# Zero rows of the routed token table: six tiles per expert written from stage 29 instead of one tile per expert after the last stage, with the first expert's weight split two stages earlier

## The chip, the cores and the metric

The kernel runs on one core of a Trainium2 chip. The metric is the device time of one execution in microseconds, 1207.06 us as the median of three runs (1206.76 to 1207.32). The core has a matrix engine (PE), two elementwise engines (DVE and ACT), a general engine (POOL) that also issues transfers, and SP, which only issues transfers. The engines meet through semaphores. Each engine runs its own instructions in the order in which they are written.

## The reference, cut to what matters

```
attn = softmax over the scores that lie within tau of the row's maximum, times v     # 4 batches x 8 heads, 576 rows, 64 columns
x    = attn as 2304 rows of 512
e    = argmax over 8 experts of cosine(x, expert_emb)
x2   = gate * (relu(x @ w1[e]) @ w2[e])                # each row by its own expert only, F = 1024
out  = softplus(x2 @ w_in) @ w_out                     # 512 -> 2048 -> 512
```

Which rows go to which expert is known only while the kernel runs, so the rows are regrouped by expert in a table in DRAM.

## The kernel before

The program has three blocks, one after the other, with a barrier of all engines between them.

**Attention** runs `stages(step)`, 36 stages numbered -1 to 34, on every engine. Stage i works on several heads at once, out of phase: in stage i PE computes the scores of head i+1 for the row maxima (`scores`), the transposed scores of head i-1 (`scores_T`), and the products with v of heads i-2 and i-1 (`values`). In stage i it also transposes the row maxima of head i (`max_T`), which the POOL makes ready in `max_lo(i)`, and the output of head i-2 (`out_T`). Each stage of a POOL program is: `write_x`, which normalises a finished head into the rows `XF` and `XR`; `q_lo` and `k_lo`, the low parts of q and k two heads ahead; `max_lo`; then the weight work of `split_first`; then the scatters. SP's stage is: q and k of head i+4, once the buffers are free, then v of head i+1 into the one of two v buffers that head i-1 has left (`sp.wait_ge(s_pv, TILES * (n - 1))`, n = i+1). SP's wait makes its stage i run while PE is already in stage i+1. The last head is 31, and its v is requested in SP's stage 30 and first read by PE in stage 32, in `values(32, 6)`, which waits on `s_vin`.

**The routed table.** After a batch's eighth head its expert choices are made (`choose_a`, `choose_b`), ranked on PE (`rank`) and turned into row numbers (`places`), and the POOL scatters the batch's 576 rows of 512 numbers into `xs_dram` with five indirect transfers. Expert e owns the rows from e*CAP on, filled from the bottom; `rt.base` is the next free row of each expert. The experts block later reads the table in tiles of 128 rows (slots), so a last, partly filled tile would read rows that nobody wrote. Hence the kernel zeroes rows. At SP's stage 2 it zeroes the 7 tiles behind the last expert. After the last stage it reads the eight final ends from `tail_row` and zeroes one tile of 128 rows from each of them (L304 to L310), then waits until all nine fills have landed, and with that the attention block ends on SP.

**The first expert's weights.** At SP's stage 4 two transfers of 2 MB fetch w1[0] and w2[0] into `first[0]` and `first[1]` (semaphore `s_e0`). At POOL's stage 7 `split_first` waits for both and issues two more transfers that copy them, converted, into the ring. In stages 9 to 12 and 16 to 19 the POOL computes the low parts, a quarter of a matrix per stage (`SPLITS`).

**The end of the block on PE** is the last `rank`, then 26 matmuls whose results nobody reads (`warm_up`).

**Experts** starts with 9 such matmuls on PE, then `x_T(0, 0)`, the transposes of the first tile, and `up(0, 0)`. The first tile is loaded by SP (L938) once all scatters have landed. ACT first computes the sums of squares of the last batch, a square root and an exponential (L1107, L1109), and then `x_hi`, the high part of the transposed tile; DVE computes the gates and then `x_lo` (L1205), for which `up` waits. From here on each tile is a slot, 25 of them, and **last_layer** follows.

Of the kernel before, what the change touches and what calls it, by code (L numbers as in the profile page):

```python
# [12 lines left out]
P = 128  # L13
B, H, S, D = 4, 8, 576, 64
# [5 lines left out]
N = B * S  # L20
DM = H * D
TT = N // P
E, F1 = 8, 1024
# [5 lines left out]
BANK = 512  # L29
# [1 line left out]
HALF = S // 2  # L31
TILES = 2 * CH
QUARTER = KD * F1
CAP = N + P
WORK = 45568


# [32 lines left out]
def warm_up(nc, out, src, times):  # L70


    for _ in range(times):
        nc.tensor.matmul(out, src[:, 0:P], src[:, 0:BANK], start=True, stop=True)

class Routing:

# [21 lines left out]
def attention(nc, sem, pb, areas, ident, XF, XR, raw, ring, first, rt, emb_en, qT, kT, v, tau, emb, moe_tau, w1, w2, xs_dram):  # L99
# [37 lines left out]
    tail_row = ar("tail_row", [1, E], I32)  # L137
    zeros = ar("zeros", [P, DM // 2], F32)
# [19 lines left out]
    sc_ps = pb("sc_ps", [P, 2 * BANK], F32)  # L158
# [14 lines left out]
    def unit(q):  # L173

        return ring[:, 0, q, :]
# [42 lines left out]
    s_tail = sem("s_tail")  # L218
    s_zero = sem("s_zero")
# [16 lines left out]
    def batch_end(b):  # L236

        return H * b + H + 2

    def batch_at(i, steps):  # L240

        b, off = divmod(i - batch_end(0) - steps, H)
        return b if off == 0 and 0 <= b < B - 1 else None
# [20 lines left out]
    with block:  # L264
        @block.sync
        def _(sp):
            sp.dma_start(emb_sb[:, :], emb).then_inc(s_emb, 16)
            for h in range(2):
                load_twice(sp, q_in[h], q_h, h, s_qin[h])
                load_twice(sp, k_in[h], k_h, h, s_kin[h])  # L270
                if h == 0:
                    sp.dma_start(tau_b[:, :], tau.partition_broadcast(P)).then_inc(s_tau, 16)
            sp.dma_start(tau2_b[:, :], moe_tau.partition_broadcast(E)).then_inc(s_tau2, 16)
            load_v(sp, v1[0], 0, s_vin[0])

            def next_q_k(i):
                n = i + 4
                if live(n):
                    sp.wait_ge(s_qlo, n - 1)
                    load_twice(sp, q_in[n % 2], q_h, n, s_qin[n % 2])  # L280
                    sp.wait_ge(s_klo, n - 1)
                    sp.wait_ge(s_kh1, n - 1)
                    load_twice(sp, k_in[n % 2], k_h, n, s_kin[n % 2])

            def step(i):
                next_q_k(i)
                n = i + 1
                if n >= 1 and live(n):
                    if n >= 2:
                        sp.wait_ge(s_pv, TILES * (n - 1))  # L290
                    load_v(sp, v1[n % 2], n, s_vin[n % 2])
                if i == 4:
                    sp.dma_start(first[0][:, :].rearrange("p (kc f) -> p kc f", f=F1),
                                 w1[0].rearrange("(kc p) f -> p kc f", p=P)).then_inc(s_e0, 16)
                    sp.dma_start(first[1][:, :].rearrange("p (kc d) -> p kc d", d=DM),
                                 w2[0].rearrange("(kc p) d -> p kc d", p=P)).then_inc(s_e0, 16)

                if i == 2:
                    sp.wait_ge(s_con, CONSTS)
                    sp.dma_start(xs_dram[E * CAP:E * CAP + (E - 1) * P, :].rearrange("(p s) (h d) -> p (s h) d", p=P, h=2),  # L300
                                 zeros[:, :].unsqueeze(1).to_broadcast([P, 2 * (E - 1), DM // 2])).then_inc(s_zero, 16)

            next_q_k(-2)
            stages(step)  # L304

            sp.wait_ge(s_tail, 1)
            for e in range(E):
                at = sp.value_load(tail_row[0:1, e:e + 1], min_val=0, max_val=E * CAP - P)
                sp.dma_start(xs_dram[bass.ds(at, P), :].rearrange("p (h d) -> p h d", h=2),
                             zeros[:, :].unsqueeze(1).to_broadcast([P, 2, DM // 2])).then_inc(s_zero, 16)  # L310
            sp.wait_ge(s_zero, 16 * (E + 1))

        @block.tensor
        def _(pe):
# [123 lines left out]
            pe.wait_ge(s_ones, 1)  # L438
            stages(step)
            rank(B - 1)  # L440
            pe.wait_ge(rt.s_w[0], 1)
            warm_up(nc, sc_ps[:, 0:BANK], unit(0), 26)

        @block.scalar
        def _(act):
# [95 lines left out]
        def _(dve):  # L541
# [86 lines left out]
            def places(b):  # L628
                dve.wait_ge(s_rk, b + 1)
                base, after = rt.base[b % 2], rt.base[(b + 1) % 2]  # L630
                nc.vector.tensor_tensor(after[:, :], rank_ps[:, CH * E:(CH + 1) * E], base[:, :],
                                        ALU.add).then_inc(s_rkr, 1)
                nc.vector.tensor_tensor(pl[:, :, :], rank_ps[:, 0:CH * E].rearrange("p (c e) -> p c e", e=E),
                                        base[:, :].unsqueeze(1).to_broadcast(wide), ALU.add).then_inc(s_rkr, 1)
                dve.wait_ge(s_rkr, 2 * (b + 1))
                link(nc.vector.tensor_tensor(pl[:, :, :], pl[:, :, :], oh[:, 0:CH, :].bitcast(F32), ALU.mult))
                link(nc.vector.reduce_sum(plf[:, :], pl[:, :, :], AX_X))
                nc.vector.tensor_copy(rt.place[:, b, :], plf[:, :]).then_inc(s_place, 1)

            def tables():  # L640
# [8 lines left out]
                link(nc.vector.reduce_sum(se[:, :], pre[:, :, :], AX_X))  # L649
                nc.vector.tensor_scalar(rt.step[:, :], nsl[:, :], -float(P), float(CAP), ALU.mult, ALU.add)  # L650
                link(nc.vector.tensor_tensor(past[:, :, :],
# [11 lines left out]
            def step(i):  # L663
                for k in range(CH):
                    row_max(i, k)
                    if k == 0:
                        rden_(i)
                    mask(i, k)
                    if i == 0 and k == 3:
                        emb_rows()  # L670
                    if i == 1 and k == 0:
                        emb_cols()
                    if k == 1 and batch_at(i, 1) is not None:
                        choose_a(batch_at(i, 1))
                    if k == 3 and batch_at(i, 1) is not None:
                        choose_b(batch_at(i, 1))
                    if k == 1 and batch_at(i, 2) is not None:
                        places(batch_at(i, 2))

            for t in kh1:  # L680
                nc.vector.memset(t[D:96, 0:S].bitcast(F32), 1.0)
# [10 lines left out]
            choose_a(B - 1)  # L692
            choose_b(B - 1)
            places(B - 1)
            nc.vector.tensor_copy(tail_row[:, :], rt.base[B % 2][0:1, :]).then_inc(s_tail, 1)
            tables()

        @block.gpsimd
        def _(pool):
# [95 lines left out]
                                        ALU.mult).then_inc(s_x, 1)  # L795

            def scatter(b, chunks):
                pool.wait_ge(s_place, b + 1)
                pool.wait_ge(s_x, X_OPS * H * (b + 1))
                for c in chunks:  # L800
                    rows = P if c < FULL else REM
                    src = XF[:, b % 2, c, :] if c < FULL else XR[0:REM, b % 2, :]
                    pool.indirect_dma_start(xs_dram, bass.IndirectOffsetOnAxis(rt.place[0:rows, b, c:c + 1], 0),
                                            src, None).then_inc(s_scat, 16)
                    scattered[0] += 1

            SPLITS = {9: (0, 0), 10: (0, 1), 11: (0, 2), 12: (0, 3), 16: (1, 0), 17: (1, 1), 18: (1, 2), 19: (1, 3)}

            def split_first(i):

                if i == 7:
                    pool.wait_ge(s_e0, 32)
                    for u in range(2):
                        pool.dma_start(unit(2 * u), first[u][:, :]).then_inc(rt.s_cast[u], 16)
                if i == 20:
                    pool.dma_start(raw[0][:, :].rearrange("p (kc f) -> p kc f", f=F1),
                                   w1[1].rearrange("(kc p) f -> p kc f", p=P)).then_inc(rt.s_raw[0], 16)
                if i in SPLITS:
                    u, c = SPLITS[i]
                    pool.wait_ge(rt.s_cast[u], 16)  # L820
                    part = QUARTER // 4
                    w = slice(c * part, (c + 1) * part)
                    ins = nc.gpsimd.tensor_tensor(unit(2 * u + 1)[:, w], first[u][:, w],
                                                  unit(2 * u)[:, w].bitcast(F32), ALU.subtract)
                    if c == 3:
                        ins.then_inc(rt.s_w[u], 1)
# [31 lines left out]
def experts(nc, sem, pb, start, ident, XF, XR, raw, ring, rt, gate, dest, w1, w2, w_in, w_out, xs_dram, ys_dram):  # L858
# [26 lines left out]
    h_ps = [pb(f"b_h{i}", [P, BANK], F32) for i in range(2)]  # L885
    ht_ps = [pb(f"b_ht{i}", [P, BANK], F32) for i in range(2)]
    y_ps = pb("b_y", [P, BANK], F32)
    wu_ps = pb("b_wu", [P, BANK], F32)
# [32 lines left out]
    with nc.Block() as block:  # L921
# [107 lines left out]
        def _(pe):  # L1029
# [48 lines left out]
                    ins = nc.tensor.matmul(y_ps[:, :], htl[:, kc, :], hi, start=False, stop=kc == KF1 - 1)  # L1078
                ins.then_inc(s_y, 1)

            warm_up(nc, wu_ps[:, :], ring[:, 0, 0, :], 9)
            x_T(0, 0)
            up(0, 0)
            pe.wait_ge(rt.s_tab, 1)
# [151 lines left out]
def last_layer(nc, sem, pb, start, ident, ring, raw, gate, dest, ys_dram, out):  # L1236
# [25 lines left out]
    h_ps = [pb(f"c_h{i}", [P, BANK], F32) for i in range(2)]  # L1262
# [42 lines left out]
    with nc.Block() as block:  # L1305
# [53 lines left out]
        def _(pe):  # L1359
# [42 lines left out]
                    ins = nc.tensor.matmul(o_ps[t][:, :], g_lo, w_hi, start=False, stop=fc == KF2 - 1)  # L1402
                ins.then_inc(s_l2, 1)

            warm_up(nc, h_ps[0][:, :], ring[:, 0, 0, :], 12)
            for c in range(FULL):
                tile_T(0, c, yg_first[:, c, :])

# [222 lines left out]
```

## Time and profile before

| | |
|---|---|
| median of three runs | 1207.06 us |
| the profiled execution | 1207.06 us, its span 1205.1 us, so 1.96 us lie outside the span |
| PE busy | 1148.0 us, 95% of the span |
| DVE, ACT, POOL busy | 49%, 45%, 39% |
| transfers of SP (queue q1) | 49.58 MB in 45376 packets |
| transfers of the POOL (queue q0) | 84.94 MB in 14496 packets |

The span is the time from the first instruction to the last. PE is the engine that is nearly always busy. PE idles mostly at the start, and at the border between attention and experts. The granted clock of PE, printed as PEclk, is 1.00 at 2.4 GHz and 0.50 at 1.2 GHz; over the span it is 0.985.

### The profile page before, as it was taken

The page shows a single profiled execution, that of the slowest core. Times are in us where ns is not written, and L with a number is a line of the kernel's source. Part 1 is how long each engine was busy: PE and PEld are TensorE (multiplying, and loading weights), DVE is VectorE, ACT ScalarE, POOL GpSimd, SP SyncE. Part 2 cuts the span into 40 slices and gives each one's busy share as a digit, 9 for nine tenths or more (in the row PEclk, how much of TensorE's full clock was granted, in tenths as well). Part 3 has the DMA queues.
Part 4 walks back from the last instruction along what each step waited for, and adds up shares of the span by engine and source line. Part 5 has one row for each costly group of instructions (what it writes and reads, how often), then busy time and mean ns, then how long its engine had stood idle before and what let it go on. Part 6 is the DMA issues. An engine that isn't in the chain of part 4 may idle for free. (4 is left out here: it accounts for less than half of the span.)

```text
span 1205.1 us, 17818 instructions
## 1 busy us (share of the span) xinstructions
PE 1148.0 (95%) x5875; PEld 939.5 (78%) x5876; DVE 586.3 (49%) x991; ACT 544.5 (45%) x997; POOL 465.8 (39%) x476
## 2 busy tenths in 40 slices
PE   3999999999999859999999999699999999999997
PEld 2888888888888647888888888578788788878886
DVE  3666676676666322221222212375565655655554
ACT  3566666656665422222222222454444544544454
POOL 4333454554333127257645566123213213223121
PEclk9999999999999969999999999999999999999999
DMA  3148413124211066776778767300000000000000
GB/s 103 51 139 267 133 51 113 50 79 150 79 51 50 10 209 242 236 255 242 267 257 313 257 234 244 123 1 27 10 35 27 9 35 17 17 35 19 1 36 18
DMA packets 59935, 135.32 MB, mean 112 GB/s; under 512 B 24280, under 2 KB 28120, under 8 KB 57056
## 3 DMA queue, kind: packets, MB, share of 16 engines
q0 software_dynamic: 14496, 84.94, 20.2%
q1 hardware_dynamic: 45376, 49.58, 13.9%
q8 instruction: 35, 0.57, 0.2%
q14 instruction: 28, 0.23, 0.1%
HBM read 76.83 MB, written 19.92 MB: 80 GB/s over the span
## 5 line engine op out<-in xcount | busy, mean ns | idle before, releaser
L1354 POOL TENSOR_TENSOR gl<-rc,gh 128x512 fp32r<-128x512 f32 (+1 forms) x80 | 92.9, 1181 | 300.5 <-ACT gh L1482 300.5
L358 PE MATMUL out_ps<-pT,v 128*66 128x288 f32 x640 | 187.1, 407 | 2.1 <-ACT oT L479 1.3
L569 DVE TENSOR_REDUCE mx<-sc_ps 128x1 f32<-128x576 f32 x160 | 121.2, 758 | 137.3 <-PE sc_ps L320 131.6
L974 POOL TENSOR_TENSOR ring<-raw,ring 128x1024 f32 (+1 forms) x64 | 151.0, 2397 | 46.3 <-DMA ring<-raw 46.1
L455 ACT ACTIVATE ering<-st_ps,esc 128x576 f32<-128x576 f32 x160 | 118.4, 740 | 45.9 <-PE st_ps L320 35.1
L579 DVE SCALAR_TENSOR_TENSOR pT<-st_ps,thr,ering 128x576 f32<-128x576 f32 x160 | 128.5, 803 | 7.4 <-ACT ering L455 7.4
L1385 PE MATMUL c_h<-c_xT,ring 128*128 128x512 f32 (+2 forms) x320 | 120.8, 377 | 3.0 <-DVE c_xT L1506 3.0
L1386 PE MATMUL c_h<-c_xT,ring 128*128 128x512 f32 (+2 forms) x320 | 120.8, 378 | 0.0
L319 PE MATMUL st_ps<-qhh,khl 128*128 128x288 f32 x320 | 119.6, 389 | 0.0
L1387 PE MATMUL c_h<-c_xT,ring 128*128 128x512 f32 (+2 forms) x320 | 119.6, 374 | 0.0
L1532 DVE TENSOR_SCALAR rc<-c_h 128x512 f32<-128x512 f32 (+1 forms) x80 | 51.0, 637 | 137.4 <-ACT ea L1469 135.8
L1400 PE MATMUL c_o<-ring,gh 128*128 128x512 f32 x288 | 115.5, 401 | 1.3 <-POOL gl L1354 1.3
L319 PE MATMUL sc_ps<-khl,qhh 128*128 128x288 f32 x320 | 96.1, 315 | 20.1 <-DVE identr L690 14.6
L1401 PE MATMUL c_o<-ring,gh 128*128 128x512 f32 x288 | 114.0, 396 | 0.0
L1402 PE MATMUL c_o<-ring,gl 128*128 128x512 f32 x288 | 114.0, 396 | 0.0
L1469 ACT ACTIVATE ea<-c_h 128x512 f32<-128x512 f32 (+1 forms) x80 | 44.4, 555 | 151.1 <-PE c_h L1387 151.1
L358 PEld LDWEIGHTS out_ps<-pT,v 128*66 128x66 f32 x640 | 83.4, 137 | 33.1 <-ACT oT L479 4.2
L1216 DVE TENSOR_TENSOR htl<-b_ht,hth 128x512 fp32r<-128x512 f32 x50 | 32.2, 686 | 131.8 <-ACT hth L1123 131.8
L320 PE MATMUL sc_ps<-khl,qlm 128*128 128x288 f32 x320 | 92.6, 303 | 0.0
L320 PE MATMUL st_ps<-qlm,kh 128*128 128x288 f32 x320 | 90.4, 297 | 0.0
L1052 PE MATMUL b_h<-ring,xth 128*128 (+1 forms) x200 | 82.6, 413 | 4.9 <-DVE xtl L1205 4.3
L1076 PE MATMUL b_y<-ring,hth 128*128 x200 | 81.2, 406 | 1.9 <-DVE htl L1216 1.9
(201 smaller groups left out, 2331.3 us busy)
## 6 DMA issues: line engine op xcount, KB each, us to landing
ring<-raw POOLq DMA_DIRECT2D x16, 2048.0 KB, 10.3
raw<-in_moe_w_dram POOLq DMA_DIRECT2D x14, 2048.0 KB, 9.6
q_in<-in_q_dram SPq DMA_DIRECT2D x64, 144.0 KB
k_in<-in_k_dram SPq DMA_DIRECT2D x64, 144.0 KB, 2.9
xs<-rows_in SPq DMA_DIRECT2D x25, 256.0 KB, 3.9
slots_out<-ys SPq DMA_DIRECT2D x25, 256.0 KB, 4.0
v<-in_v_dram SPq DMA_DIRECT2D x32, 128.0 KB
first<-in_moe_w_dram SPq DMA_DIRECT2D x2, 2048.0 KB, 11.6
```

Source lines behind the costliest of these rows:

```text
L319: nc.tensor.matmul(out[:, h, :], stat1[:, w], mov1[:, m], start=True, stop=False)
L320: ins = nc.tensor.matmul(out[:, h, :], stat2[:, w], mov2[:, m], start=False, stop=True)
L358: nc.tensor.matmul(out_ps[0:VW, 0:HALF], v1[n % 2][:, c, :], pT[n % 2][c][:, h * HALF:(h + 1) * HALF], start=c == 0, stop=c == CH - 1).the ...
L455: nc.scalar.activation(flat(ering[b]), halves(st_ps[b]), ACT.Exp, scale=esc[:, :]).then_inc(s_e, 1)
L569: nc.vector.reduce_max(mx[n % 2][:, c:c + 1], halves(sc_ps), AX_XY).then_inc(s_max, 1)
L579: nc.vector.scalar_tensor_tensor(out=flat(pT[n % 2][c]), in0=halves(st_ps[t % 2]), scalar=thr[:, :], in1=flat(ering[t % 2]), op0=ALU.is_ge ...
L974: ins = nc.gpsimd.tensor_tensor(ring[:, bass.ds(side, 1), 2 * u + 1, w].rearrange("p o w -> p (o w)"), raw[u][:, w], ring[:, bass.ds(side, ...
L1385: nc.tensor.matmul(h_ps[fc % 2][:, 0:n], w_hi, x_hi, start=kc == 0, stop=False)
L1386: nc.tensor.matmul(h_ps[fc % 2][:, 0:n], w_hi, x_lo, start=False, stop=False)
L1387: ins = nc.tensor.matmul(h_ps[fc % 2][:, 0:n], w_lo, x_hi, start=False, stop=kc == KD - 1)
L1400: nc.tensor.matmul(o_ps[t][:, :], g_hi, w_hi, start=fc == 0, stop=False)
L1401: nc.tensor.matmul(o_ps[t][:, :], g_hi, w_lo, start=False, stop=False)
```

## The change

- `CAP`, the rows that each expert owns, goes from 2432 to 3 * 576 + 6 * 128 = 2496, so the tables' addresses shift.
- `tail_row` is now copied from `rt.base` after batch 2's places (in DVE's stage 28), and holds where batch 3 will begin for each expert. In SP's stage 29, behind the load of head 30's v, eight fills of 768 rows each (1536 pieces of 1 KB, 1.57 MB per fill, 12.58 MB in all) are issued. They cover whatever rows batch 3 will take (at most 576) and one tile beyond. The eight fills of 128 rows after the last stage are gone, the final wait for all nine stays.
- Since batch 3's rows are now written over zeroed rows, the POOL waits for the fills before it scatters batch 3.
- The 26 unread matmuls at the end of attention are gone, and those at the start of experts go from 9 to 24.
- `split_first` waits for `s_e0` and issues its two transfers in stage 5 instead of 7; the quarters are computed in stages 7 to 12 and 16, 17.

```diff
-CAP = N + P
+TAIL = 6
+CAP = 3 * S + TAIL * P
...
+                if i == batch_end(B - 2) + 3:
+
+                    sp.wait_ge(s_tail, 1)
+                    for e in range(E):
+                        at = sp.value_load(tail_row[0:1, e:e + 1], min_val=0, max_val=E * CAP - TAIL * P)
+                        sp.dma_start(xs_dram[bass.ds(at, TAIL * P), :].rearrange("(p s) (h d) -> p (s h) d", p=P, h=2),
+                                     zeros[:, :].unsqueeze(1).to_broadcast([P, 2 * TAIL, DM // 2])).then_inc(s_zero, 16)
...
-            sp.wait_ge(s_tail, 1)
-            for e in range(E):
-                at = sp.value_load(tail_row[0:1, e:e + 1], min_val=0, max_val=E * CAP - P)
-                sp.dma_start(xs_dram[bass.ds(at, P), :].rearrange("p (h d) -> p h d", h=2),
-                             zeros[:, :].unsqueeze(1).to_broadcast([P, 2, DM // 2])).then_inc(s_zero, 16)
             sp.wait_ge(s_zero, 16 * (E + 1))
...
-            pe.wait_ge(rt.s_w[0], 1)
-            warm_up(nc, sc_ps[:, 0:BANK], unit(0), 26)
...
+                        if batch_at(i, 2) == B - 2:
+                            nc.vector.tensor_copy(tail_row[:, :], rt.base[(B - 1) % 2][0:1, :]).then_inc(s_tail, 1)
...
-            nc.vector.tensor_copy(tail_row[:, :], rt.base[B % 2][0:1, :]).then_inc(s_tail, 1)
...
             def scatter(b, chunks):
+                if b == B - 1:
+                    pool.wait_ge(s_zero, 16 * (E + 1))
...
-            SPLITS = {9: (0, 0), 10: (0, 1), 11: (0, 2), 12: (0, 3), 16: (1, 0), 17: (1, 1), 18: (1, 2), 19: (1, 3)}
+            SPLITS = {7: (0, 0), 8: (0, 1), 9: (0, 2), 10: (0, 3), 11: (1, 0), 12: (1, 1), 16: (1, 2), 17: (1, 3)}
...
-                if i == 7:
+                if i == 5:
                     pool.wait_ge(s_e0, 32)
...
-            warm_up(nc, wu_ps[:, :], ring[:, 0, 0, :], 9)
+            warm_up(nc, wu_ps, ring[:, 0, 0, :], 24)
```

What stands in a row on SP around the end of attention. The numbers behind `v` tell its two buffers apart; the last `v_79` is head 31's. Before:

```order
L259 DMA v_78<-in_v_dram 128x4x64 [waits s_pv]
L261 DMA v_78<-in_v_dram 64x64
L259 DMA v_79<-in_v_dram 128x4x64 [waits s_pv]
L261 DMA v_79<-in_v_dram 64x64
L308 TENSOR_LOAD tail_row [waits s_tail]
L308 ISA x2
L309 ISA
L309 DMA rows_in<-zeros 256x1x256
```

Of the eight fills after the change, the first and the last are shown:

```order
L260 DMA v_78<-in_v_dram 128x4x64 [waits s_pv]
L262 DMA v_78<-in_v_dram 64x64
L307 TENSOR_LOAD tail_row [waits s_tail]
L307 ISA x2
L308 ISA
L308 DMA rows_in<-zeros 1536x1x256
...
L308 DMA rows_in<-zeros 1536x1x256
L260 DMA v_79<-in_v_dram 128x4x64 [waits s_pv]
L262 DMA v_79<-in_v_dram 64x64
L265 UNCONDITIONAL_BRANCH [waits s_zero]
```

All eight fills now stand ahead of the load of head 31's v on the one queue.

On the POOL, around the copies of the first expert's weights. `mt<-mx` is `max_lo`, `khl` the end of `k_lo`. Before, in stages 6 and 7:

```order
L773 TENSOR_TENSOR mt<-mx_116,mt 128x5 [waits s_mhi]
L765 TENSOR_TENSOR khl_131<-k_in_74,khl_131 64x576 [waits s_mt,s_qlo,s_khi]
L788 TENSOR_TENSOR LP_88<-os_82,rden_114 128x5x8 [waits s_rd,s_klo]
L790 TENSOR_TENSOR XF<-os_82,rden_114 128x4x64
L793 TENSOR_TENSOR XR<-os_82,rden_114 64x64
L751 TENSOR_TENSOR qlm_128<-q_in_73,qhh_124 128x576 [waits s_qhh]
L773 TENSOR_TENSOR mt<-mx_117,mt 128x5 [waits s_mhi]
L765 TENSOR_TENSOR khl_132<-k_in_75,khl_132 64x576 [waits s_mt,s_qlo,s_khi]
L814 DMA ring<-first_69 128x4096 [waits s_e0,s_klo]
L814 DMA ring<-first_70 128x4096
```

After, at the end of stage 5 and in stage 6:

```order
L774 TENSOR_TENSOR mt<-mx_117,mt 128x5 [waits s_mhi]
L766 TENSOR_TENSOR khl_134<-k_in_75,khl_134 64x576 [waits s_mt,s_qlo,s_khi]
L817 DMA ring<-first_69 128x4096 [waits s_e0,s_klo]
L817 DMA ring<-first_70 128x4096
L789 TENSOR_TENSOR LP_88<-os_83,rden_115 128x5x8 [waits s_rd]
L791 TENSOR_TENSOR XF<-os_83,rden_115 128x4x64
L794 TENSOR_TENSOR XR<-os_83,rden_115 64x64
L752 TENSOR_TENSOR qlm_127<-q_in_72,qhh_123 128x576 [waits s_qhh]
L774 TENSOR_TENSOR mt<-mx_116,mt 128x5 [waits s_mhi]
```

The wait for `s_e0` moved from behind stage 7's `max_lo` to ahead of stage 6's.

On PE, at the border of the blocks, before:

```order
L412 MATMUL tr_ps<-oh,ones_sq 128x8
L74 MATMUL sc_ps<-ring 128x512 [waits s_w0]
L74 MATMUL sc_ps<-ring 128x512 x25
L264 UNCONDITIONAL_BRANCH
L1028 UNCONDITIONAL_BRANCH [waits barrier_Pool_Activation_PE_DVE_SP_release]
L74 MATMUL b_wu<-ring 128x512 x9
L1036 MATMUL b_tr<-ident,xs_6229 128x128 [waits s_xs0]
```

and after:

```order
L414 MATMUL tr_ps<-oh,ones_sq 128x8
L265 UNCONDITIONAL_BRANCH
L1031 UNCONDITIONAL_BRANCH [waits barrier_Pool_Activation_PE_DVE_SP_release]
L75 MATMUL b_wu<-ring 128x512 x24
L1039 MATMUL b_tr<-ident,xs_6203 128x128 [waits s_xs0]
```

The unread matmuls now all stand behind the barrier.

## Rows read from the trace of the kernel before

**Rows 1.** Busy time by stretch: from:to, length, engines, PEclk, DMA share, GB/s.
```profile
50.00:373.00 323.00, 322.92 (x2042) 271.30 (x2041) 210.03 (x330) 208.94 (x398) 140.97 (x182) 1.00 0.37 106
```

**Rows 2.** Order of time: start, us, engine, line, operation [idle before <-releaser]. The border.
```profile
422.73 0.17 DVE L638 CAST place<-plf 128x5 int32<-128x5 f32 x1
423.18 1.03 POOL L803 DMA_INDIRECT rows_in<-XF,place  x1 [3.87 <-DVE place L638]
423.97 11.54 SPq L309 DMA_DIRECT2D rows_in<-zeros  x8
428.31 0.90 POOL L803 DMA_INDIRECT rows_in<-XR,place  x1 [0.30 <-issue]
437.86 4.18 PE L74 MATMUL b_wu<-ring 128*128 128x512 f32 x9 [8.00 <-PEq L264]
```

**Rows 3.** Order of time, SP around its stage 4.
```profile
86.65 0.59 SPq L293 DMA_DIRECT2D first<-in_moe_w_dram  x1
87.28 0.51 SPq L295 DMA_DIRECT2D first<-in_moe_w_dram  x1
92.34 1.18 SPq L256 DMA_DIRECT2D k_in<-in_k_dram  x2
```

**Rows 4.** The tile `first`: from issue to landing of SP's two transfers.
```profile
DMA to landing us min/median/max: 8.4/11.6/14.8
```

**Rows 5.** The tile `k_in`: to landing, those issued at 92.34, then those of 76.12.
```profile
DMA to landing us min/median/max: 10.4/10.7/11.1
...
DMA to landing us min/median/max: 2.8/2.9/3.0
```

**Rows 6.** Order of time, POOL's stages 5 to 7.
```profile
85.48 1.43 POOL L765 TENSOR_TENSOR khl<-k_in,khl 64x576 fp32r<-64x576 f32 x1 [0.17 <-POOL mt L773]
...
93.91 0.26 POOL L788 TENSOR_TENSOR LP<-os,rden 128x40 f32<-128x40 f32 x1 [7.00 <-DVE rden L591]
...
96.98 0.20 POOL L773 TENSOR_TENSOR mt<-mx,mt 128x5 fp32r<-128x5 f32 x1 [0.61 <-ACT mt L463]
...
110.98 1.35 POOL L814 DMA_DIRECT2D ring<-first  x2 [0.31 <-POOL khl L765]
```

**Rows 7.** Order of time, PE: max_T of stage 6.
```profile
99.17 0.77 PE L374 MATMUL tr_ps<-identr,mt 128*128 128x128 f32 x4
```

**Rows 8.** Busy time by stretch: during the fill issued at 62.91, the loads of `first`, the border.
```profile
65.00:66.00 1.00, 1.00 (x8) 0.79 (x7) 0.41 (x1) 0.95 (x3) 0.00 (x0) 1.00 1.02 351
66.00:67.00 1.00, 1.00 (x10) 0.84 (x8) 1.00 (x2) 0.05 (x1) 0.00 (x0) 1.00 1.04 347
...
90.00:95.00 5.00, 5.00 (x35) 4.34 (x34) 2.80 (x6) 3.28 (x6) 1.09 (x4) 1.00 1.01 372
...
430.00:436.00 6.00, 0.00 (x0) 0.00 (x0) 0.00 (x0) 0.00 (x0) 0.00 (x0) 0.73 0.69 217
```

**Rows 9.** Order of time, SP: v of head 30, then of head 31.
```profile
385.79 0.37 SPq L259 DMA_DIRECT2D v<-in_v_dram  x1
386.21 0.52 SPq L261 DMA_DIRECT2D v<-in_v_dram  x1
...
397.18 0.37 SPq L259 DMA_DIRECT2D v<-in_v_dram  x1
```

**Rows 10.** Order of time, PE: values(32, 6) and what follows, and the 26 unread matmuls.
```profile
407.76 1.16 PE L358 MATMUL out_ps<-pT,v 128*66 128x288 f32 x4
...
420.72 1.21 PE L412 MATMUL tr_ps<-oh,ones_sq 128*128 128x40 f32 x5
421.78 8.08 PE L74 MATMUL sc_ps<-ring 128*128 128x512 f32 x26
```

**Rows 11.** PE by stretch: length, PE busy (instructions), PEclk, DMA share, GB/s.
```profile
419.00:420.00 1.00, 0.00 (x0) 0.53 0.00 0
...
425.00:426.00 1.00, 1.00 (x4) 0.55 0.93 341
426.00:427.00 1.00, 1.00 (x6) 1.00 0.88 314
...
453.00:454.00 1.00, 1.00 (x6) 0.90 1.18 475
```

**Rows 12.** Order of time, start of experts.
```profile
445.27 0.58 ACT L1113 ACTIVATE xth<-b_tr 128x512 fp32r<-128x512 f32 x1
446.43 0.68 DVE L1205 TENSOR_TENSOR xtl<-b_tr,xth 128x512 fp32r<-128x512 f32 x1
447.16 0.80 PE L1052 MATMUL b_h<-ring,xth 128*128 128x512 f32 x1 [4.26 <-DVE xtl L1205]
```

More of the change, by code:

```diff
@@ L73, in warm_up @@
     for _ in range(times):
-        nc.tensor.matmul(out, src[:, 0:P], src[:, 0:BANK], start=True, stop=True)
+        nc.tensor.matmul(out[:, :], src[:, 0:P], src[:, 0:BANK], start=True, stop=True)
 class Routing:
@@ L1403, in second @@
                 ins.then_inc(s_l2, 1)
-            warm_up(nc, h_ps[0][:, :], ring[:, 0, 0, :], 12)
+            warm_up(nc, h_ps[0], ring[:, 0, 0, :], 12)
             for c in range(FULL):
```

## The prediction

> **What bounds the kernel now.** I read the busy time by stretch first. Through attention PE is busy 322.92 us of 323 [rows 1], so whatever holds PE there is added to the time in full; no other engine can win it back. Then I read the order of time at the border of attention and experts. The last batch's row numbers are ready at 422.90, the POOL's five scatters run from 423.18 to 429.21, but experts start only at 437.86, and PE idles 8.00 us [rows 2]. What ends last there is SP, whose eight fills are issued over 11.54 us from 423.97 and must land. This is what the change takes away. Last I looked at where the moved work goes: SP's and POOL's rows around stage 4 to 7 and stage 29 to 32 [rows 3 to 7, 9, 10], and the rates of the transfers [rows 8].
>
> **Part 1: the POOL's wait in stage 5.** SP issues the two 2 MB loads of `first` at 86.65 and 87.28 [rows 3]. They land 8.4 and 14.8 us later [rows 4], the second at 87.28 + 14.8 = 102.1. Before, the POOL asks at 110.98 [rows 6] and waits for nothing. After, it asks when stage 5's `k_lo` is done, at 85.48 + 1.43 = 86.9, and stands until 102.1. Queued behind it on the POOL are the two copies (0.3 to start and 1.35, [rows 6]) and stage 6: from the start of `LP` at 93.91 to the start of `mt` at 96.98 it is 3.07 us, of which 0.61 was waiting, so 2.46 of work, then 0.20 for `mt`, and 0.3 to get going. `mt` is then done at 102.1 + 1.65 + 0.3 + 2.46 + 0.20 = 106.7, where it was 97.18. PE needs it for `max_T` at 99.17 [rows 7] and is held 7.5 us; everything behind on PE (the scores, the products) waits too.
>
> PE has then been idle that long, and the clock matters. In the rows the granted clock falls to 0.53 in the slice 419 to 420, after idle time, and after work has started again (PE's row at 420.72, the rank's matmuls) it is back at 1.00 only from about 425.9; from the start at 447.16 it stays low until about 453.2 [rows 10 to 12]. That is 5.2 to 6.0 us at 1.2 GHz instead of 2.4, of which about half is lost where PE is the bound: I take 2.7 us. Part 1 costs 7.5 + 2.7 = 10.2 us. Its lower end is 7.5, should the other engines' waits hide the slow clock; its upper end 11.
>
> The copies now run beside the loads of q and k for head 10, as they ran beside those of head 11; that collision cost PE nothing before (the whole of rows 1), so 0, at most 2 if ACT is caught. The quarters of `SPLITS` are the same eight instructions, in stages where the POOL idles 7.00 us [rows 6]: 0. They and the weights are ready by stage 17, long before they are used: 0. The new `CAP` changes only addresses: 0.
>
> **Part 2: the fills on SP's queue.** The first fill follows head 30's v, whose second load ends its issue at 386.21 + 0.52 = 386.73 [rows 9]. `tail_row` has been ready since stage 28, so SP doesn't wait. A fill of the same form (pieces of 1 KB) moves 351 and 347 GB/s in whole microseconds [rows 8]; 12.58 MB take 12.58 / 0.349 = 36.0 us. Batch 2's last three scatters (0.66 MB) share the engines, 1.9 us. With 1.3 us until the first bytes flow, the fills end at 386.73 + 1.3 + 36.0 + 1.9 = 425.9.
>
> Behind them in the queue stands head 31's v, issued at 397.18 before [rows 9]. That SP's queue works in order shows at stage 4: the small `k_in` loads issued at 92.34, behind the 4 MB, took 10.4 to 11.1 us to land, against 2.8 to 3.0 without such a load ahead [rows 5]; they landed 1.2 us after `first`. So v lands at about 425.9 + 0.4 + 1.2 = 427.5. PE wants it at 407.76 [rows 10] and is held 19.7 us, and after that it runs slow for a while, again 2.7. For the fill rate I keep both ends: 372 GB/s, as the load of `first` [rows 8], makes the hold 2.2 us shorter, and 314 GB/s, the slice 426 to 427 [rows 11] with fills and scatters mixed, 4.1 us longer.
>
> The Trainium skill ("DMA: Bandwidth & Descriptors", "Where 436 GB/s comes from") gives about 358 GB/s as what a core gets of the DRAM. By that figure the fill would take 35.1 us and the time would be 0.9 us less. The 372 GB/s of the stretch 90 to 95 [rows 8] go past it, so I leave it out of the sum.
>
> **Part 3: the border.** All of it moves by 19.7 + 2.7 = 22.4. The last scatter's issue ends at 428.31 + 0.90 + 22.4 = 451.6. The fills are then long in, so the wait that the POOL has been given is free, and SP has only the wait for them left, also done. With 0.3 for the barrier experts start at 451.9, against 437.86: +14.0 (without the hold it would be 429.5, and this part would win 8.3).
>
> At the start of experts, PE now has 24 unread matmuls. The 26 took 8.08 us [rows 10], low until 425.9 and full after: 0.43 and 0.24 us each fit that. From an idle start, 5.3 us low do 12 of them, the other 12 take 2.9, together 8.2 us. ACT's path to `xth` takes 445.27 - 437.86 = 7.4 us [rows 2, 12], and the first tile must wait for the scatters' landing and its own load, which I put at 5 to 6 us, so the unread matmuls are now what ends last. Then come four transposes (0.6), `xth` 0.58, `xtl` 0.68 and the handovers, 2.1 in all: `up` starts 10.3 us into the block, against 447.16 - 437.86 = 9.3 [rows 12]: +1.0. In return `up` finds the clock high: the low stretch from 447.16 to 453.2 is gone, -2.7 (taken as above; 0 if the short idle time before `up` lets the clock fall again).
>
> **The sum.** 10.2 + 14.0 + 1.0 - 2.7 = +22.5 us. Later PE is the bound again and the POOL's weight copies move with the block, so nothing more is won or lost. The profiled execution took 1207.06 us (1205.1 span and 1.96 around it), which is also the median: 1229.6 us, with a span near 1227.6. Its own range is 1222 to 1238: down by 2.2 for the rate, 2.7 for the clock in part 1 and 2.7 more for part 2's, up by 4.1 and by 2.7 and 2 for the clock and ACT.
>
> **The rivals.**
>
> *Head 31's v isn't late.* Its transfer overtakes the fills. For it: it is a separate, small transfer. Against: the landing times [rows 5]. Then only the POOL waits, for the fills until about 427 instead of starting at 423.18: the border moves 3.8 later than without them, experts start at 433.3, `up` at 443.6, -3.6 and -2.7 for the clock, +10.2 of part 1: 1211.0. In the Trainium skill ("DMA: Bandwidth & Descriptors", "Queues, rings and completion order") completion is not in order per issuing engine, but each ring's entries are taken in order; that lends this rival little.
>
> *The wait in stage 5 doesn't reach PE.* Part 1 is 0, the rest stays: 1219.4. Against it: PE needs `mt` 2.0 us after the POOL has it [rows 6, 7], and the POOL is 15.2 us late.
>
> *The shorter border decides.* The place is the end of SP's work at 437.86, its price up to -8.3, +1.0 and -2.7, -10.0 in all, and it decides as long as what the two queues hold PE is less than 10.0 us together. With no hold on PE and only the POOL's wait of 3.8, the time is 1200.8. For it: this stretch holds 8.00 us of idle PE [rows 2], surely on the path. Against: part 1 alone uses it up.
>
> *The fills run slower than I think.* Eight small fills moved only 217 GB/s in 430 to 436 [rows 8]. At that rate 12.58 MB take 58.0 us, 22.0 more: 1251.6. Against: those were bound by their issue, 1.5 us for each 256 KB, and the large fill was not.
>
> **Chances.** My forecast 0.75; v in time 0.07; stage 5 hidden 0.06; the shorter border 0.04; slow fills 0.08. The range 1210 to 1244 leaves out the last two. A change of 0.2%, 2.4 us, is about what a measurement of this kernel can tell from none. Faster by more than that comes from the fourth case: 0.04, and 0.01 for what I haven't thought of; same 0.02, between the cases; slower 0.93.
>
> **What the profile after would show.** Part 1: POOL idle for about 15 us from 86.9, ended by the landing of `first`, PE idle 7.5 us before the `max_T` that stood at 99.17, then the clock at half for 5 to 6 us. Part 2: SP's issue of the fills drawn out over some 30 us, and PE idle about 20 us before a `values` matmul, ended by the landing of v; PEclk low behind it. Part 3: no idle SP time between the last scatter and the barrier, 24 matmuls over 8.2 us, and `up` at full clock. I am wrong if PE doesn't wait for v, or if the transfers in that stretch stay well off 349 GB/s.

## The result and the profile after

The changed kernel takes 1234.35 us (median of four runs, 1233.67 to 1235.82), the kernel before 1206.91: ratio 1.0228, interval 1.021 to 1.0246, so 27.4 us slower. The forecast was 1229.6. The profiled execution took 1232.68 us with a span of 1230.8, which is 25.7 us more than the span before; the comparison below is of these two.

What PE waited for in the changed kernel, longest first (engine, line, waited for: us in total, times, longest):

```profile
PE out_ps L360 <- DMA v<-in_v_dram: 21.6, 1, 21.6
PE sc_ps L321 <- DVE identr L692: 14.7, 1, 14.7
PE b_wu L75 <- PEq L265: 10.7, 1, 10.7
PE tr_ps L376 <- POOL mt L774: 6.4, 1, 6.4
```

The first and the fourth are new. The second is the program's start, the third the border between the blocks, which was 8.0 long before [rows 2]. The same two holds in order of time (start, duration, engine, and in brackets the wait before it):

```profile
85.14 1.43 POOL L766 TENSOR_TENSOR khl<-k_in,khl 64x576 fp32r<-64x576 f32 x1 [0.17 <-POOL mt L774]
101.58 1.35 POOL L817 DMA_DIRECT2D ring<-first  x2 [15.01 <-DMA first<-in_moe_w_dram]
...
105.39 0.19 POOL L774 TENSOR_TENSOR mt<-mx,mt 128x5 fp32r<-128x5 f32 x1
...
105.63 1.12 PE L376 MATMUL tr_ps<-identr,mt 128*128 128x128 f32 x4 [6.42 <-POOL mt L774]
...
394.66 0.52 SPq L262 DMA_DIRECT2D v<-in_v_dram  x1
396.46 30.66 SPq L308 DMA_DIRECT2D rows_in<-zeros  x8
427.16 4.54 SPq L260 DMA_DIRECT2D v<-in_v_dram  x1
437.69 2.16 PE L360 MATMUL out_ps<-pT,v 128*66 128x288 f32 x4 [21.56 <-DMA v<-in_v_dram]
```

The POOL stands 15.01 us behind its `k_lo`, its `mt` comes at 105.39 instead of 96.98 [rows 6], and `max_T` at 105.63 instead of 99.17 [rows 7]. SP stands in the issue of the eight fills for 30.66 us (the first two of them alone take 2.04 us in e5_spread below), and v is requested only at 427.16 instead of 397.18 [rows 9]. PE's `values(32, 6)` starts at 437.69 instead of 407.76 [rows 10].

The border of the blocks, in order of time:

```profile
452.41 1.21 PE L414 MATMUL tr_ps<-oh,ones_sq 128*128 128x40 f32 x5
460.49 0.90 POOL L806 DMA_INDIRECT rows_in<-XR,place  x1 [0.30 <-issue]
464.35 7.75 PE L75 MATMUL b_wu<-ring 128*128 128x512 f32 x24 [10.73 <-PEq L265]
...
471.94 0.60 PE L1039 MATMUL b_tr<-ident,xs 128*128 128x128 f32 x4
473.95 0.50 PE L1055 MATMUL b_h<-ring,xth 128*128 128x512 f32 x1 [1.41 <-DVE xtl L1208]
```

The last scatter's issue ends at 461.39, and yet experts start only at 464.35. The rows of the barrier's line say why: what each queue did there (operation, duration in ns, start). Changed kernel:

```profile
L265 SPq DRAIN  x1: 7/7/7, 437.1 to 437.1; - x1
L265 PEldq DRAIN  x1: 1477/1477/1477, 452.2 to 452.2; - x1
L265 POOLq DRAIN  x1: 7041/7041/7041, 457.0 to 457.0; - x1
```

and before:

```profile
L264 POOLq DRAIN  x1: 10645/10645/10645, 423.0 to 423.0; - x1
L264 SPq DRAIN  x1: 7/7/7, 437.6 to 437.6; - x1
```

In both kernels experts start 0.2 to 0.3 us after the last of these drains has ended. The POOL's drain (its row starts at 457.03) ends at 464.1, 2.7 us behind its last issue. Before it ended at 433.6, and SP, at 437.6, was later by 4.0.

Last, PE around the end of experts, by stretch (length, PE busy, PEclk, DMA share, GB/s). Changed:

```profile
784.00:786.00 2.00, 1.24 (x5) 1.00 0.43 159
786.00:788.00 2.00, 2.00 (x6) 0.52 0.00 0
788.00:790.00 2.00, 2.00 (x7) 0.63 0.00 0
```

Before:

```profile
760.00:762.00 2.00, 0.82 (x4) 1.00 0.57 217
762.00:764.00 2.00, 2.00 (x10) 1.00 0.06 12
```

Behind the same idle time of 1.88 us (PE waits for `htl` there in both) the clock falls to half for about 3 us in one and not in the other.

| place | before | changed | later by |
|---|---|---|---|
| max_T of stage 31 | 398.51 | 406.94 | 8.4 |
| rank (its ones_sq matmuls) | 420.72 | 452.41 | 31.7 |
| experts start | 437.86 | 464.35 | 26.5 |
| up starts | 447.16 | 473.95 | 26.8 |
| first hidden transposes | 456.63 | 480.71 | 24.1 |
| last hidden transposes | 758.26 | 781.84 | 23.6 |
| last layer starts | 770.26 | 795.39 | 25.1 |
| end | 1205.1 | 1230.8 | 25.7 |

### The profile page after: what moved, and what is told of

It is laid out like the page before. It is cut to its first block and busy times, and to the rows that moved or that the text cites. A ratio compares the mean times of both kernels' runs of the same rounds, so it can differ in the third digit from the quotient of the medians.

```text
span 1230.8 us, 17795 instructions
## 1 busy us (share of the span) xinstructions
PE 1146.4 (93%) x5864; PEld 937.6 (76%) x5865; DVE 585.5 (48%) x991; ACT 545.1 (44%) x997; POOL 466.2 (38%) x476
## 5 line engine op out<-in xcount | busy, mean ns | idle before, releaser
L360 PE MATMUL out_ps<-pT,v 128*66 128x288 f32 x640 | 189.2, 411 | 23.5 <-DMA v<-in_v_dram 21.6
L789 POOL TENSOR_TENSOR LP<-os,rden 128x40 f32<-128x40 f32 x32 | 8.2, 255 | 198.3 <-DVE rden L591 198.2
```

The source lines that it names most:

```text
L360: nc.tensor.matmul(out_ps[0:VW, 0:HALF], v1[n % 2][:, c, :], pT[n % 2][c][:, h * HALF:(h + 1) * HALF], start=c == 0, stop=c == CH - 1).the ...
```

## The experiments

The theory: two queues hold PE, one after the other. The POOL stands in stage 5 until `first` has landed, and v stands in SP's queue behind 12.58 MB of fills. The rivals are that slack hides the first, that the load on the 16 transfer engines rather than the order in the queue holds v, and that the number of the fills, not their bytes, costs the time.

**e1_split_only**, the kernel before with the weight work moved and nothing else:

```diff
-SPLITS = {9: (0, 0), 10: (0, 1), ... 19: (1, 3)}
+SPLITS = {7: (0, 0), 8: (0, 1), 9: (0, 2), 10: (0, 3), 11: (1, 0), 12: (1, 1), 16: (1, 2), 17: (1, 3)}
-                if i == 7:
+                if i == 5:
                     pool.wait_ge(s_e0, 32)
```

> The kernel before with only the move of the first expert's weight work: the wait for s_e0 and the two copies in stage 5 instead of 7, the quarters in stages 7 to 12 and 16, 17. Theory (the POOL stands until the second load of first has landed, and PE behind it): POOL idle about 15 us, PE held 6.5 to 7 us before max_T of stage 6, then some 5 us at half clock that cost 2 more, so +8.8 us on the kernel before, 1215.7. Rival (the hold is taken up by slack in later stages and the loss of the changed kernel is all in the fills): +0 to +3 us, under 1210.

Measured: 1216.99 us, ratio 1.0082 (1.0066 to 1.0099), so 10.3 more than the kernel before. In its trace the POOL stands 15.55 us, PE waits once for `mt`:

```profile
PE tr_ps L374 <- POOL mt L773: 7.0, 1, 7.0
```

`max_T` of stage 31 is 9.9 us late (408.39), and the end of experts shows the slow clock again (13.5 us from the last transposes to the last layer, 12.0 before). The hold in stage 5 reaches PE, and later stages don't make up for it. The rival falls.

**e2_old_split**, the changed kernel with that move undone (the diff above, reversed).

> The changed kernel with the wait for s_e0, the copies and the quarters back in their old stages; fills, row capacity and unread matmuls stay changed. Theory (the two holds on PE are separate and add up): 8.8 us less than the changed kernel's 1234.35, so 1225.5, with PE still held 21 to 22 us for head 31's v. Rival (the hold in stage 5 shifts something that the fills would otherwise hit anyway, so that the holds overlap): less than 5 us gained, over 1229.

Measured: 1224.14 us, ratio 1.0146 (1.0129 to 1.0163). The wait for v is as long as in the changed kernel, and the one for `mt` is gone from PE's list:

```profile
PE out_ps L360 <- DMA v<-in_v_dram: 21.5, 1, 21.5
```

The parts add up: 10.3 + 17.4 = 27.7 against 27.4 for both.

**e3_v_on_act**, the changed kernel with head 31's v issued from ACT's queue:

```diff
+                        if i == HEADS - 1:
+                            load_v(act, v1[i % 2], i, s_vin[i % 2])     # ACT's stage, behind out_copy(i, 1)
...
-                if n >= 1 and live(n): ... load_v(sp, v1[n % 2], n, s_vin[n % 2])
+                (the same for n < HEADS - 1 only)
```

> The changed kernel, but the two transfers of head 31's v are issued from ACT's own queue, in its stage 31 behind the out_copy that already waits for the same buffer to be free. Theory A (v was late because it stood behind 12.58 MB in SP's queue): v is issued near 406 and lands within 3 to 14 us (k_in took 13.4 us beside the POOL's copies), PE is held 0 to 4 us at values(32, 6) instead of 21.6. Then the POOL's new wait decides: the row numbers are ready near 431, the fills land near 437, so the scatters start 18 us earlier than in the changed kernel: about 1216. Theory B (the 16 transfer engines are full, and whichever queue v is in it lands only when the fills are through): PE held about 20 us, 1232 to 1235.

Measured: 1216.59 us, ratio 1.0077 (1.0054 to 1.01). In order of time, ACT's issue and the POOL's first scatter:

```profile
405.89 0.44 ACTq L260 DMA_DIRECT2D v<-in_v_dram  x1
406.37 1.60 ACTq L262 DMA_DIRECT2D v<-in_v_dram  x1
...
437.04 1.03 POOL L809 DMA_INDIRECT rows_in<-XF,place  x1 [8.25 <-DMA rows_in<-zeros]
```

PE doesn't wait for v at all, though all eight fills are under way beside it (SP issues them over 30.70 us from 396.73, as in the changed kernel). So it was the order in one queue, not the load of the engines. The other expected wait takes its place: the POOL idles 8.25 us until the fills have landed, the last 4.7 of them with the row numbers ready (`place` is done at 432.38). The Trainium skill ("DMA: Bandwidth & Descriptors", "Issuing engines are not separate DMA queues") says that transfers of different issuers run on the same 16 engines and interleave, and that several issuers save only issue time. The trace agrees with the interleaving. It doesn't agree that only issue time is at stake: for this one small transfer the choice of the issuer was worth 17.8 us of the kernel's time, since on SP the fills stood ahead of it.

**e4_three_tiles**, half the bytes per fill (the upper three tiles of each expert's range aren't zeroed):

```diff
-xs_dram[bass.ds(at, TAIL * P), :] ... [P, 2 * TAIL, DM // 2]
+xs_dram[bass.ds(at, 3 * P), :] ... [P, 2 * 3, DM // 2]
```

> The changed kernel with fills of 3 tiles (384 rows) instead of 6, so 6.29 MB in all. It leaves out the zeroing of the upper three tiles of each expert's range; with these inputs batch 3 gives no expert that many rows. Theory (the hold is the fills' bytes over their rate, 341 GB/s in the changed kernel): fills through 18.4 us earlier, v lands near 419.5, PE held about 3.5 us instead of 21.6, and most of the slow clock behind it goes too: 1215 to 1217. Rival (the hold is mostly issue cost on SP, eight issues with their register reads, whatever their size): still held over 12 us, over 1225.

Measured: 1213.66 us, ratio 1.0071 (1.0049 to 1.0093). The hold, in order of time:

```profile
395.91 14.31 SPq L308 DMA_DIRECT2D rows_in<-zeros  x8
410.26 2.55 SPq L260 DMA_DIRECT2D v<-in_v_dram  x1
418.56 1.16 PE L360 MATMUL out_ps<-pT,v 128*66 128x288 f32 x4 [2.97 <-DMA v<-in_v_dram]
```

Half the bytes take 18.6 us off the hold, 6.29 MB at 338 GB/s. The same eight issues with the same register reads cost PE at most these 2.97 us. The time is a little better than expected; the hold was 0.5 us shorter than the 3.5 put for it. The clock does fall behind it, but not for long: it reads 0.50 in 420 to 422 and 0.84 in 422 to 426.

**e5_spread**: with what was learned, the fills are spread so that at most two stand between two loads of v, and the weight work is back in its stages:

```diff
-                if i == batch_end(B - 2) + 3:
+                FILLS = {batch_end(B - 2) + 2: (0, 1), batch_end(B - 2) + 3: (2, 3), batch_end(B - 2) + 4: (4, 5, 6, 7)}
+                if i in FILLS:
                     sp.wait_ge(s_tail, 1)
-                    for e in range(E):
+                    for e in FILLS[i]:
```

> The changed kernel with the first expert's weight work back in its old stages, and the eight fills split over three of SP's stages: experts 0 and 1 in stage 28, 2 and 3 in stage 29, 4 to 7 in stage 30, each time behind that stage's load of v. Theory (fills cost time only by standing ahead of v, 4.6 us for each 1.57 MB): at most two fills, 9.2 us, stand between one v and the next, 11.9 us later, the last four end near 418, before the row numbers at 422.9; no hold. The last scatter is issued by 429.2, the POOL's drain ends 2.7 us later, experts start near 432.1 instead of 437.9, up starts at 441.7 at full clock: 8 us less than the kernel before, 1198.7 (1197.5 to 1200). Rival (12.58 MB of writes beside attention and the scatters cost time wherever they are): no faster than 1205.

Measured: 1200.94 us, ratio 0.9956 (0.9943 to 0.9968): faster than the kernel before, by 5 us instead of 8. In order of time:

```profile
388.22 2.04 SPq L308 DMA_DIRECT2D rows_in<-zeros  x2
396.67 0.39 SPq L260 DMA_DIRECT2D v<-in_v_dram  x1
...
399.15 10.38 SPq L308 DMA_DIRECT2D rows_in<-zeros  x4
...
422.87 1.02 POOL L806 DMA_INDIRECT rows_in<-XF,place  x1 [4.05 <-DVE place L638]
...
431.86 8.34 PE L75 MATMUL b_wu<-ring 128*128 128x512 f32 x24 [10.74 <-PEq L265]
...
442.05 0.50 PE L1055 MATMUL b_h<-ring,xth 128*128 128x512 f32 x1 [1.41 <-DVE xtl L1208]
448.81 1.06 PE L1064 MATMUL b_ht<-ident,hr 128*128 128x128 f32 x8 [0.44 <-DVE hr L1214]
...
456.78 0.66 PE L1039 MATMUL b_tr<-ident,xs 128*128 128x128 f32 x4 [0.36 <-DMA xs<-rows_in]
```

The border is as expected: no hold, experts start at 431.86, the first hidden transposes are 7.8 us earlier than at 456.63 before. But the next tile lands late (PE waits for `xs`, which it didn't before), and the second hidden transposes come at 463.48 against 470.12, only 6.6 earlier; and behind the last ones this execution has the slow clock, 13.55 us against 12.0. That leaves 5.1. The 12.58 MB beside attention cost nothing visible (the last rank's `ones_sq` matmuls start at 420.12, before at 420.72), so the rival falls too.

**e6_spread_9**, the same with `warm_up(nc, wu_ps, ring[:, 0, 0, :], 9)` for 24.

> As e5_spread, with 9 unread matmuls at the start of experts instead of 24. Theory (24 keep PE busy until the first tile is there and bring the clock up; 9 leave it idle and the clock falls again): up starts 0.3 us earlier but runs some 6 us at half clock: 2.2 to 2.7 us slower than e5_spread. Rival (the unread matmuls only delay the first transposes): 0.3 us faster than e5_spread.

Measured: 1202.41 us, ratio 0.9964 (0.9951 to 0.9977). The intervals overlap, so the medians decide nothing. The traces do in part: `up` starts at 441.75 instead of 442.05 and runs slow, so the first hidden transposes are at 450.00 instead of 448.81. From the second on, 463.56 against 463.48, nothing is left of it: e5_spread waits for the late tile there, and here PE, 1.2 us later, finds it landed. What 24 unread matmuls win here is lost one slot later.

**e7_stage6**, e5_spread with the weight work one stage earlier than before:

```diff
-                if i == 7:
+                if i == 6:
-SPLITS = {9: (0, 0), ... 12: (0, 3), 16: (1, 0), ... 19: (1, 3)}
+SPLITS = {8: (0, 0), 9: (0, 1), 10: (0, 2), 11: (0, 3), 12: (1, 0), 16: (1, 1), 17: (1, 2), 18: (1, 3)}
```

> As e5_spread, with the wait for s_e0 and the copies in stage 6, the quarters in stages 8 to 12 and 16 to 18. Theory (the POOL's wait costs PE only what it makes the next max_lo late): the POOL reaches the wait near 98.8, stands until about 102.1, has the copies issued by 103.8, before stage 7's LP at 105.8: PE isn't held and the time is e5_spread's within 1 us. Rival (the copies beside the loads of q and k for head 10 are what held PE): PE held and 3 us or more slower than e5_spread.

Measured: 1201.33 us, ratio 0.9959 (0.9946 to 0.9971), the same as e5_spread. The POOL waits, and PE doesn't:

```profile
102.30 1.35 POOL L817 DMA_DIRECT2D ring<-first  x2 [3.60 <-DMA first<-in_moe_w_dram]
105.66 0.25 POOL L789 TENSOR_TENSOR LP<-os,rden 128x40 f32<-128x40 f32 x1 [2.01 <-DVE rden L591]
```

The POOL still has 2.01 us to spare before stage 7's `LP`. The copies are issued at 102.30, close to the 101.58 of the changed kernel and the 102.64 of e1_split_only, and PE isn't held, so it was the POOL's lateness and not the copies' traffic. (The match isn't perfect: here q and k for head 10 are requested before the copies, at 98.44 and 99.79, and there behind them, at 105.44 and 107.80. But there PE had stopped by 99.2 and 99.7, before the copies began.)

**e8_last_slot** and **e9_before_last**: seven unread matmuls in the idle time before the last `down_`, on e7_stage6 and on the kernel before.

```diff
             slot(SLOTS - 1, 0, last=True)
+            warm_up(nc, wu_ps, xth[:, :, :].rearrange("p k t -> p (k t)"), 7)
             down_(SLOTS - 1, expert_of(SLOTS - 1))
```

> As e7_stage6, with 7 more unread matmuls (source xth) on PE between the last transposes of experts and the last down_, where PE idles 1.9 us for DVE's htl. In the traces so far the time from those transposes to the first matmul of the last layer is 12.0 us in some executions and 13.55 in others, the clock at half for about 3 us behind that idle time in the latter. Theory (the short idle time sometimes takes the clock down, so two executions of one kernel differ by 1.5 us): always 12.0 to 12.2, the median 0 to 1.2 us under e7_stage6's 1201.3 and the spread of the runs (3.9 us there) smaller. Rival (the fall comes from elsewhere, such as the transfers running then): 13.5 can still be seen in the trace and the spread stays.

> The kernel before with the same 7 unread matmuls ahead of the last down_ and nothing else. Theory: 0 to 1 us under the kernel before. Rival: the matmuls themselves delay down_ and it is up to 1 us slower.

Measured: e8 1199.66 us, ratio 0.9945 (0.9932 to 0.9959), the fastest kernel here; e9 1206.34, ratio 0.9998 (0.9989 to 1.0007), no difference. In both traces the stretch is short; e8's rows in order of time:

```profile
750.01 1.03 PE L1064 MATMUL b_ht<-ident,hr 128*128 128x128 f32 x8
750.80 1.86 PE L75 MATMUL b_wu<-xth 128*128 128x512 f32 x7
...
762.03 5.46 PE L75 MATMUL c_h<-ring 128*128 128x512 f32 x12 [3.23 <-PEq L924]
```

12.02 us, and 12.1 in e9. But four kernels without the seven also had 12.0 (before, e2, e4 and e7), the runs of e8 still spread over 2.7 us (3.9 for e7) and those of e9 over 2.3 (2.4 for the kernel before beside it), and e8's interval overlaps that of e7. So the short stretch is in line with the theory, but a gain isn't shown.

## Why the prediction was right, step by step

**The mechanisms and their order** were as forecast: POOL held 15 us in stage 5, PE behind it, PE held some 20 us for v, the POOL's new wait free, the border shorter. The measured time lies inside the likeliest case's own range (1222 to 1238). Forecast +22.5, median +27.4, profiled spans +25.7. That the total came so close is luck in part: by the spans the single terms missed by -1.8, +0.9, +3.1, -0.7 and +1.6, and some of it cancels. The sizes, by the spans:

- **Part 1**, forecast 7.5 + 2.7 = 10.2. Measured 8.4 (6.5 until `max_T`, 2.0 for the clock). The hold is shorter because `first` landed at 100.9 instead of 102.1: SP asked 0.3 us sooner, and the landing took 14.0 us instead of 14.8. That isn't shown to be an effect of the change: the landing took 14.0 to 14.5 us in the four kernels in which the POOL stops in stage 5, and 13.7 to 14.8 in the others. In e1_split_only the landing took 14.5, and the two parts were 7.5 and 2.4.
- **Part 2**, forecast 19.7 + 2.7 = 22.4. Measured 31.7 - 8.4 = 23.3, of it 21.6 of waiting and 1.7 for the clock. The fills started 1.3 us later than put, as SP reads its register first, and ran at 334 GB/s over the stretch, not 349:

```profile
396.00:436.00 40.00, 19.74 (x119) 15.61 (x118) 11.22 (x17) 12.49 (x25) 3.98 (x9) 0.81 1.02 334
```

The Trainium skill ("DMA: Bandwidth & Descriptors", "Where 436 GB/s comes from") gives about 358 GB/s as a core's share of the DRAM. This rate stays below it, as do e4's 338.

- **Part 3, the start of experts**: this term was mis-sized. I took 0.3 us for the barrier and a win of 8.3. The barrier came 3.0 us behind the last scatter's issue, as the POOL's drain ends 2.7 us behind it. The win was 5.2. In the kernel before, the drain ended at 433.6, hidden behind SP; I had looked only at what ended last, not at what would be next.
- **Part 3, the unread matmuls**, forecast +1.0 and -2.7. Measured +0.3 (24 took 7.6 until the first transposes, not 8.2) and -2.7. The +0.3 is of this one trace: `up` starts 10.2 and 10.4 us into the block in e5_spread and e7_stage6, where the forecast has 10.3.
- **"Nothing more is won or lost"** was wrong by +1.6: half a microsecond won in the second slot, 1.5 us lost to the clock at the last `down_`, 0.6 at the start of the last layer. The first of the losses isn't shown to be the change's: kernels with the fills and the 24 matmuls show 12.0 or 13.5 us there, and so does the kernel before with the weight work moved alone (13.5).

The remaining 1.7 us between the median and the profiled execution isn't explained; that execution was faster than all four timed runs.

**The rivals**: v in time was refuted as an event and shown as a possibility (e3). That stage 5 doesn't reach PE was refuted by e1. The shorter border did not decide in the changed kernel; with both holds gone it does (e5). The fills weren't slow (334 GB/s, not 217).

## What to carry to other kernels

A transfer moved to "where the queue is idle" moves ahead of everything that its queue carries next: count its bytes over the measured rate, and compare with the time until the first consumer behind it, and if that is too long, split it between those loads or use another queue. A wait put into an engine's program is paid by whoever waits for the next thing that this engine makes, here PE, two stages from any weight. When you take away what ends last at a barrier, look up when each other queue was done before you count the win.

## What the hardware showed that I hadn't expected

- The POOL's drain at the end of attention ended 2.7 us behind the issue of its last scatter in every kernel whose fills were over by then (the changed kernel and e2 to e8), and 4.4 us behind it in the kernel before, where fills ran beside it (4.0 in e1, 4.1 in e9). At the very end of the program, where the POOL's last work is elementwise, its drain ends 1.5 us behind that work.
- An idle time of 1.9 us on PE, with the same work around it, was followed by a stretch at half clock, worth 1.5 us, in five of the nine traces without the seven unread matmuls, and by none in the other four. What decides it isn't shown.
